# Earlier row loads, inverse matrices on semaphores of their own, and a reordered first wave in a spectral mixing and gated feed-forward kernel

## The reference

```python
X = np.fft.rfft(x, axis=1)                    # x: 4 x 3008 x 256
Yr = Xr @ w_r - Xi @ w_i + b_r
Yi = Xr @ w_i + Xi @ w_r + b_i
Yr, Yi = soft_threshold(Yr, 0.01), soft_threshold(Yi, 0.01)
y = np.fft.irfft(Yr + 1j * Yi, n=3008, axis=1)
h = y.reshape(12032, 256) @ w_in              # d_ff = 2048
P = a[0] + a[1]*h + a[2]*h**2 + a[3]*h**3
Q = 1 + abs(b[0])*abs(h) + abs(b[1])*h**2
out = (P / (Q + 1e-6)) @ w_out
```

## Time and profile before

| | us |
|---|---|
| median of 3 runs | 1527.56 |
| lowest and highest of them | 1527.35, 1531.04 |
| the profiled execution, its own time | 1528.65 |
| its span | 1526.9 |
| PE busy in the span | 1452.5 (95%) |
| DVE busy | 1273.0 (83%) |
| ACT busy | 1216.0 (80%) |
| POOL busy | 635.9 (42%) |

### The profile page before, as it was taken

One profiled execution on the slowest core, in us unless ns is written; L12 is line 12 of the kernel. 1 busy time (PEld: TensorE's weight loads), 2 busy tenths in 40 slices (PEclk: granted clock), 3 DMA queues, 4 the chain that ended last, 5 costly groups with the idle time before them and its releaser, 6 DMA issues.

```text
span 1526.9 us, 19941 instructions
## 1 busy us (share of the span) xinstructions
PE 1452.5 (95%) x6976; PEld 1231.3 (81%) x6976; DVE 1273.0 (83%) x1301; ACT 1216.0 (80%) x1577; POOL 635.9 (42%) x420
## 2 busy tenths in 40 slices
PE   6888999999999999999999999999999999999986
PEld 2666788888888888888888888888888778887775
DVE  0242888888888888889899899889999999999997
ACT  3454887888887887888888888888888888888886
POOL 0000344444444444444444444444455555555554
PEclk9999999999999999999999999999999999999999
DMA  8945565655655655555555564565455544555443
GB/s 262 285 131 153 106 141 114 151 127 122 137 129 111 145 128 114 133 112 115 111 125 102 116 128 94 115 128 114 88 120 113 102 89 102 110 107 101 95 78 69
DMA packets 97570, 187.90 MB, mean 123 GB/s; under 512 B 11104, under 2 KB 57504, under 8 KB 97472
## 3 DMA queue, kind: packets, MB, share of 16 engines
q0 software_dynamic: 29952, 98.58, 35.2%
q1 hardware_dynamic: 67520, 88.05, 20.0%
HBM read 50.54 MB, written 37.49 MB: 58 GB/s over the span
## 4 chain that ended last, share of the span: by engine, by line
PE 62%; DVE 21%; DMA 7%; issue 6%; ACT 2%; SPq 1%; POOL 1%; POOLq 0%; ACTq 0%
PE h_ps L359 20%; PE o_ps L372 7%; PE o_ps L384 7%; PE o_ps L374 7%; DVE num L642 5%; DVE g_hi L634 5%; DVE den L637 5%; DVE num L617 4%; PE d L332 4%; PE d L333 4%; DMA zp_in<-spec 3%; PE d L344 3%; PE d L338 2%; DMA inv_in<-in_inv 2%; PE d L319 2%
## 5 line engine op out<-in xcount | busy, mean ns | idle before, releaser
L661 POOL TENSOR_TENSOR g_lo<-num,sq 128x940 fp32r<-128x940 f32 (+1 forms) x208 | 453.5, 2180 | 260.5 <-DVE num L642 260.2
L652 POOL DMA_DIRECT2D den<-sq x208 | 182.5, 877 | 624.5 <-ACT sq L506 314.8
L372 PE MATMUL o_ps<-g_hi,wout_hi 128*128 128x470 f32 (+1 forms) x832 | 330.2, 398 | 0.0
L359 PE MATMUL h_ps<-yt_hi,win_hi 128*128 128x470 f32 (+1 forms) x832 | 312.5, 376 | 4.4 <-DVE num L622 3.0
L359 PE MATMUL h_ps<-yt_lo,win_hi 128*128 128x470 f32 (+1 forms) x832 | 312.0, 375 | 0.0
L359 PE MATMUL h_ps<-yt_hi,win_lo 128*128 128x470 f32 (+1 forms) x832 | 310.0, 373 | 0.0
L374 PE MATMUL o_ps<-g_hi,wout_lo 128*128 128x470 f32 (+1 forms) x832 | 309.1, 372 | 0.0
L384 PE MATMUL o_ps<-g_lo,wout_hi 128*128 128x470 f32 (+1 forms) x832 | 227.5, 395 | 30.1 <-POOL g_lo L661 29.9
L506 ACT ACTIVATE sq<-h_ps,bsq 128x940 f32<-128x940 f32 (+1 forms) x208 | 214.7, 1032 | 50.3 <-POOL g_lo L661 50.1
L503 ACT ACTIVATE den<-h_ps,b_sb 128x940 f32<-128x940 f32 (+1 forms) x208 | 213.8, 1028 | 48.3 <-PE h_ps L359 47.5
L642 DVE SCALAR_TENSOR_TENSOR num<-num,a_sb,den 128x940 f32<-128x940 f32 (+1 forms) x208 | 245.6, 1181 | 5.0
(11 more groups left out here) (64 smaller groups left out, 1492.1 us busy)
## 6 DMA issues: line engine op xcount, KB each, us to landing
den<-sq POOLq DMA_DIRECT2D x200, 470.0 KB, 4.4
xw<-in_x SPq DMA_DIRECT2D x32, 384.0 KB, 4.3
spec<-s1w SPq DMA_DIRECT2D x64, 192.0 KB, 3.3
z_in<-spec SPq DMA_DIRECT2D x96, 128.0 KB, 3.2
spec<-s_out SPq DMA_DIRECT2D x96, 128.0 KB, 3.3
out_t<-o_sb SPq DMA_DIRECT2D x25, 470.0 KB, 5.6
zp_in<-spec SPq DMA_DIRECT2D x22, 480.0 KB, 5.0
inv_in<-in_inv SPq DMA_DIRECT2D x96, 64.0 KB, 2.3
```

Of the source, the lines that this page charges most:

```text
L359: mm = pe.matmul(h_ps[q % 2][:, j, 0:cols(q)], w[:, h, f * P:(f + 1) * P], y[t % 2][:, h, 0:cols(q)], start=i == 0, stop=i == len(terms) - 1)
L372: pe.matmul(o_ps[:, h, 0:w], wout_hi[:, f, h * P:(h + 1) * P], g_hi[q % 2][:, j, 0:w], start=f == 0, stop=False)
L661: pool.tensor_tensor(g_lo[r % 2][:, :, 0:cols(r)], ring(num, r), ring(sq, r), ALU.mult).then_inc(n_g, 1)
```

## The change

It does six things.

1. `s_z` now counts row loads alone; the inverse matrices have semaphores `s_inv` of their own, on which s4 waits. `load_z` waits for `p2` (the s2 that last used the row buffer) in place of `p4`; a new `load_inv` waits for `p4`.
2. In the wave, SP at u loads the rows of step u+4 ahead of its stores (before: of step u+2, behind them), and the inverse of step u+2 behind its store.
3. In the start, the first x load is split in two halves with a semaphore `s_first` for the first half. The x loads 10 and 11, `fwd_sb` part 0, `wr_sb`, `wi_sb` and the bias no longer stand between the s1 stores; they come behind the 16th store, and the last three behind the first four row loads. PE waits for them at its first s3, not ahead of the wave.
4. The 12 s1 steps of batch 1 move from iterations 0 to 11 to the iterations in `EARLY_S1`, their x loads to `EARLY_X`.
5. The weight loads move from iterations 1 to 8 to every second one from 6 to 20; `weight_hi` and `weight_lo` start four iterations later.
6. s5 of tile 0 moves from behind the wave into iteration 27, its `group_f1(0)` into iteration 28, ahead of the last s4. `load_zp(1)` moves from slot 1 of the main loop to ahead of it. In the main loop the rows are loaded two slots earlier relative to their step.

```diff
+EARLY_S1 = {u: S1N + 4 + i for i, u in enumerate((4, 5, 7, 8, 9, 11, 12, 13, 15, 16, 17, 18))}
+EARLY_X = {u: S1N // 2 + 3 + i for i, u in enumerate((3, 5, 8, 11, 14))}
...
                 if c >= 4:
+                    sp.wait_ge(p2, c - 3)
+                load(z_in[c % 4][:, :], spec1[n, k2 * 4:(k2 + 1) * 4, :].rearrange("r (p d) -> (r p) d", d=D), s_z[c % 4])
+
+            def load_inv(c):
+                if c >= 4:
                     sp.wait_ge(p4, c - 3)
...
+                load(inv_in[c % 4][:, :], inv[c % K2], s_inv[c % 4])
...
+                if u < PRE and u + 4 < PRE + 4:
+                    load_z(u + 4)
...
                 if u >= 2:
                     store_s4(u - 2)
-                    if u + 2 < PRE + 4:
-                        load_z(u + 2)
-                if 1 <= u <= 8:
-                    load_weight(u - 1)
+                    load_inv(u + 2)
+                if u % 2 == 0 and 6 <= u < 22:
+                    load_weight(u // 2 - 3)
...
+                    if u == 1:
+                        pe.wait_ge(s_wc, 16 * 3)
...
+                if u == PRE - 1:
+                    pe.wait_ge(e1, 2 * S1N)
+                    pe.wait_ge(s_ff, 16)
+                    step_s5(0, o_ps[:, 0, :])
+                    step_s5(1, o_ps[:, 1, :])
+                if u == PRE:
+                    pe.wait_ge(w_lo, 8)
+                    pe.wait_ge(e2, 2 * PRE)
+                    group_f1(0)
```

More of the change, by code:

```diff
@@ L100, in z_slot @@
 def z_slot(c):
-    old = S2_SLOTS[c - 4 - PRE] + 3 if c - 4 >= PRE else 0
+    old = S2_SLOTS[c - 4 - PRE] + 1 if c - 4 >= PRE else 0
     n = c // K2
@@ L110 @@
     Z_AT.setdefault(z_slot(_c), []).append(_c)
+INV_AT = {(S2_SLOTS[_c - 4 - PRE] + 3 if _c - 4 >= PRE else 0): [] for _c in range(PRE + 4, NK)}
+for _c in range(PRE + 4, NK):
+    INV_AT[S2_SLOTS[_c - 4 - PRE] + 3 if _c - 4 >= PRE else 0].append(_c)
 def done_by(table, q, before):
@@ L163, in spectral_ffn @@
         s_w = [sem(f"s_w{i}") for i in range(8)]
+        s_first = sem("s_first")
         s_x = [sem(f"s_x{i}") for i in range(4)]
         s_z = [sem(f"s_z{i}") for i in range(4)]
+        s_inv = [sem(f"s_inv{i}") for i in range(4)]
         s_zp = [sem(f"s_zp{i}") for i in range(2)]
@@ L218, in load_z @@
                 if c >= 4:
+                    sp.wait_ge(p2, c - 3)
+                load(z_in[c % 4][:, :], spec1[n, k2 * 4:(k2 + 1) * 4, :].rearrange("r (p d) -> (r p) d", d=D), s_z[c % 4])
+            def load_inv(c):
+                if c >= 4:
                     sp.wait_ge(p4, c - 3)
-                load(z_in[c % 4][:, :], spec1[n, k2 * 4:(k2 + 1) * 4, :].rearrange("r (p d) -> (r p) d", d=D), s_z[c % 4])
-                load(inv_in[c % 4][:, :], inv[k2], s_z[c % 4])
+                load(inv_in[c % 4][:, :], inv[c % K2], s_inv[c % 4])
             def load_fwd(i):
@@ L259, in _ @@
             load(c1_sb[:, :], c1, s_tc)
-            load_x(0)
+            load(x_in[0][:, 0:2, :].rearrange("r p d -> r (p d)"), x[0, :, 0:2 * D], s_first)
+            load(x_in[0][:, 2:4, :].rearrange("r p d -> r (p d)"), x[0, :, 2 * D:4 * D], s_x[0])
             load(a_sb[:, :], coef_a, s_coef)
@@ L266, in _ @@
                 store_s1(g)
-                if g % 2 == 1:
+                if g % 2 == 1 and g // 2 + 4 < S1N // 2 + 2:
                     load_x(g // 2 + 4)
[L269 to L273, removed]
+            load_fwd(0)
             for c in range(4):
                 load_z(c)
-            for u in range(PRE + 2):
[L277 to L281, removed]
+            load(wr_sb[:, :, :], w_r.rearrange("(h p) e -> p h e", p=P), s_wc)
+            load(wi_sb[:, :, :], w_i.rearrange("(h p) e -> p h e", p=P), s_wc)
+            load(bias_sb[:, :], bias, s_wc)
+            load_inv(0)
+            load_inv(1)
+            load_x(S1N // 2 + 2)
+            load_inv(2)
+            load_inv(3)
+            for u in range(PRE + 2):
                 if u < 3:
@@ L285, in _ @@
                     load_zp(0)
+                if u < PRE and u + 4 < PRE + 4:
+                    load_z(u + 4)
+                if u == 0:
+                    for g in range(S1N, S1N + 4):
+                        store_s1(g)
+                if u - 1 in EARLY_S1:
+                    store_s1(EARLY_S1[u - 1])
+                if u in EARLY_X:
+                    load_x(EARLY_X[u])
                 if u >= 2:
                     store_s4(u - 2)
-                    if u + 2 < PRE + 4:
-                        load_z(u + 2)
-                if 1 <= u <= 8:
-                    load_weight(u - 1)
+                    load_inv(u + 2)
+                if u % 2 == 0 and 6 <= u < 22:
+                    load_weight(u // 2 - 3)
                 if u == 9:
                     load(c5_sb[:, :], c5, s_ff)
+            load_zp(1)
             for k in range(S1N, S1N + 4):
@@ L301, in _ @@
                     load_z(c)
+                for c in INV_AT.get(q, []):
+                    load_inv(c)
                 if q - 1 in S1_AT:
@@ L306, in _ @@
                         load_x(g // 2 + 4)
-                if q % SLOTS == 1 and q // SLOTS + 1 < NT:
+                if q % SLOTS == 1 and 1 <= q // SLOTS < NT - 1:
                     load_zp(q // SLOTS + 1)
@@ L316, in step_s1 @@
             def step_s1(g, bank):
-                pe.wait_ge(s_x[g // 2 % 4], (g // 8 + 1) * 16)
+                if g == 0:
+                    pe.wait_ge(s_first, 16)
+                else:
+                    pe.wait_ge(s_x[g // 2 % 4], (g // 8 + 1) * 16)
                 at = g % 2 * 2
@@ L322, in step_s2 @@
             def step_s2(c, bank):
-                pe.wait_ge(s_z[c % 4], (c // 4 + 1) * 32)
+                pe.wait_ge(s_z[c % 4], (c // 4 + 1) * 16)
                 for h in range(KH):
@@ L336, in step_s4 @@
             def step_s4(c, bank):
+                pe.wait_ge(s_inv[c % 4], (c // 4 + 1) * 16)
                 pe.wait_ge(m_thr, c + 1)
@@ L392, in _ @@
                 step_s1(g, o_ps[:, g % 2, :])
-            pe.wait_ge(s_wc, 16 * 3)
             for u in range(PRE + 2):
@@ L408, in _ @@
                     step_s4(u - 2, (d0, d1)[u % 2][:, :])
-                g = S1N + 4 + u
-                if g < 2 * S1N:
+                if u in EARLY_S1:
+                    g = EARLY_S1[u]
                     pe.wait_ge(e1, g - 1)
                     step_s1(g, o_ps[:, g % 2, :])
[L413 to L418, removed]
+                if u == PRE - 1:
[7 more added lines that the diff above has]
+                    group_f1(0)
             pe.wait_ge(m_t, PRE)
-            group_f1(0)
             group_f1(1)
@@ L521, in _ @@
                     below(u - 1)
-                g = S1N + 4 + u
-                if g < 2 * S1N:
+                if u in EARLY_S1:
+                    g = EARLY_S1[u]
                     evacuate_s1(g, o_ps[:, g % 2, :])
[L525 to L528, removed]
+                if 10 <= u < 26 and u % 2 == 0:
+                    weight_hi((u - 10) // 2)
+                if u == PRE - 1:
+                    evacuate_s5(0, o_ps[:, 0, :])
+                    evacuate_s5(1, o_ps[:, 1, :])
             act.wait_ge(w_lo, 8)
@@ L606, in _ @@
                 shifted(u - 1, h_ps[1][:, (u - 1) % 2, :])
-                if 7 <= u < 23 and u % 2 == 1:
-                    weight_lo((u - 7) // 2)
+                if 11 <= u < 27 and u % 2 == 1:
+                    weight_lo((u - 11) // 2)
                 soft(u - 1)
-            split_lo(0, o_ps[:, 0, :])
-            split_lo(1, o_ps[:, 1, :])
+                if u == PRE - 1:
+                    split_lo(0, o_ps[:, 0, :])
+                    split_lo(1, o_ps[:, 1, :])
             for q in range(NS + 1):
```

## The result

The changed kernel takes 1515.84 us (median of 5 runs, 1513.61 to 1518.10) against 1527.56 (by now the median of 5 runs too, 1526.08 to 1531.04): ratio 0.992, 95% interval 0.9903 to 0.9938. It is faster by 11.7 us where 21.8 were forecast, and lies outside the range of 1501 to 1513.

A forecast was written before the change was run, and what follows sets the result against it. The prediction took row reloads to bound the wave and the DMA queue the start. Start, wave and end terms put group 0 at 127.3 for 149.09, 21.8 us less: 1506.85 from 1528.65, about 1506 against the median; range 1501 to 1513.

The forecast's parts named there:

- From there both kernels run the same: ACT, DVE, then f1(2): From ACT's begin of group 0, forecast at 127.3 for 149.09 us, both kernels were to run the same.
- The main loop I cost at nothing: Main loop: rows go out in the same odd slots, PE's own matmuls hide them, so no time was added.
- s3(0) after 36: Start: a sign that the forecast is wrong, PE's first s3 coming after 36 us.
- First row load near 28: Start: a sign that the forecast is right, SP's first row load at 28.2 for 32.43 us.
- s3(0) at 33.7: Start: PE begins its first s3 at 33.7 for 38.42 us, bounds 33.1 to 35.9, a gain of 4.7 us.
- for completion: Start: some 0.7 us added after the queue has moved 1.57 MB by 32.8, giving 33.5 us.
- The wave: First s3 to the end of iteration 27: 79.9 us of PE work, plus 1.5 for cover and 2.6 for low clock.
- the 1.5 us for the short cover: Wave: the chain s3, bias, neg, ythr, s4 has one iteration of cover, nearly closed without an s1; 1.5 us (0 to 5).
- (b): Rival, wave: the DMA queue binds; some 22 MB at only 220 GB/s take 100 us, 10 more: 1516 us; chance 0.13.
- (c): Rival, wave: the row load was not the limit; only start and end gain, 4.7 and 1.7 us: 1521 us; chance 0.04.
- s5 late by 1.6: End of the wave: s5 waits 1.6 us (0 to 4) for zp_in, whose load waits for the store of s4(23).
- rival (a): Low clock stays: group_f1(0) takes 4.37 us, and a second s3 and a half run low: 1510 us; chance 0.11.

The follow-up runs named there:

- before_late_x2: The kernel before with load_zp(1) and x loads 16 to 19 made to wait for group_f1(0), some 2.6 us ahead of the first den DMA: 1535.31 us.
- x_half2: The changed kernel with x loads 18 and 19 (786 KB) moved from ahead of the main loop to its slots 2 and 3: 1513.52 us.
- x_zp2: The changed kernel with x loads 16 to 19 issued right behind load_zp(0) in iteration 26: 1507.93 us.
- tail_undone2: The changed kernel with s5 of tile 0 and group_f1(0) behind the whole wave again, SP's order unchanged: 1511.03 us.
- x_early2: The changed kernel with x loads 16 to 19 issued in iterations 21 to 24 of the wave instead of behind it: 1513.62 us.

## Why the prediction was wrong

The step that failed is "From there both kernels run the same: ACT, DVE, then f1(2)", with "The main loop I cost at nothing". They did not run the same: the first `den` DMA took 11.1 us for 4.5, and 6.5 us were lost behind group 0. Without them the 4.2 us by which group 0 was late would have left the time inside the range. Two of the signs named for a wrong forecast came: s3(0) after 36, and a main loop longer by more than 2 us. Point by point, for the profiled execution (1517.63 measured, 1506.85 forecast, 10.8 us apart):

- **First row load near 28: right**, 28.80.
- **s3(0) at 33.7: 36.48, 2.8 late**, and beyond the bound of 35.9. The first row load went out 0.6 us later than forecast (28.80 for 28.2), and so the bias, at 31.61. It then took 4.8 us to land, where the forecast left it 2.7 (from 31.0 to 33.7). In the four other profiles with this start s3(0) came at 33.65 to 34.66, near the forecast, but by luck: there the rows went out at 26.90 to 27.51, earlier than forecast, and the bias took 3.7 to 4.9 us. The term that was too small is the landing of the bias. Of its parts, the 0.7 us "for completion" stand in no row.
- **The wave: right.** From s3(0) to the end of iteration 27 it took 82.4 us for 84.0. The low clock behind the wait for the bias cost 2.8 us for 2.6 (from 36.48 to 41.1 the granted clock was 0.50), and the 1.5 us for the short cover were not needed. Without an s1 an iteration takes 2.60 us in the chain. s2 waited for rows once, 1.8 us, in iteration 0. The reload of the rows was the limit, and rivals (b) and (c) are refuted: the wave moved 232 GB/s and ran out of nothing.
- **s5 late by 1.6: 3.0 late**, since the store ahead took 2.67 us for the 1.78 between store and load in the earlier trace rows, and the load 4.68 for 4.3.
- **The low clock at the end, rival (a), came in part.** s5 took 3.01 for 2.22 at a granted clock of 0.78, and s3(27) with s4(26) 3.29 for 2.16 at 0.68, together 1.9 us more; `group_f1(0)` itself ran at 1.00, in 2.56. With all that, and 0.3 won at ACT's copy, group 0 began at 131.48 for 127.3, 4.2 late. Rival (c) gave the end of the wave 1.7 us, but the forecast's own terms make it 2.8 (149.09 - 136.73 against 127.3 - 117.7).
- **The rest: 1384.3 for 1377.8 us, 6.5 lost.** 4.2 and 6.5 are the 10.7 of the spans.

What the runs showed in the place of the failed step: the order of PE decides when SP's queue is let go. I had followed the waiting store on SP and asked who needs the loads behind it ("needed two slots later"), but not which other DMA is in flight when they all go at once. The cause is shown from three sides. Put into the kernel before, where nothing else changes, it costs 6.0 us by slot 4 (before_late_x2). Fewer bytes shorten `den` in step, 11.1, 7.9 and 4.8 us for 2.06, 1.28 and 0.49 MB issued just ahead of it or beside it (changed, x_half2, x_zp2). And taken out by moving four loads, it gives back 7.9 us of median (x_zp2); in the profiles the rest gives 7.4.

The Trainium skill has the rule, on the page "DMA: Bandwidth & Descriptors", section "Issuing engines are not separate DMA queues": DMAs started by SP and by GpSimd run on the same 16 engines and interleave. The trace agrees: POOL's DMA took 11.1 us while SP's five loads moved, and 4.5 without them.

As for the parts: 1 and 2 alone bring 17.6 us. Part 6 (s5 and f1 inside the wave) is worth about 3 us when no collision stands in the way: 1507.93 with it (x_zp2) against 1511.03 without it (tail_undone2), whose x loads do not collide either. The two also differ in where the x loads stand. The forecast had given the end of the wave about 2.8. In the change as made, part 6 brought the collision and cost 4.8 us net. Parts 3, 4 and 5 together brought nothing that could be told apart: 1511.03 with them and without part 6, 1510.42 without. Their gain at s3(0), 4.5 us in the profiles, was there, and in tail_undone2 it was spent again. 2.2 us went in the wave (82.6 for 80.4), which began at a granted clock of 0.50 after a wait of 3.3 us for the bias. 2.5 us went at its end, where the last s4 waited 2.3 us behind a late store and s5 ran 4.42 us for 3.08, at a granted clock of 0.50. Whether part 5 alone does anything was not tried.

## What to carry to other kernels

When a wait is moved on an in-order queue, list everything queued behind it that will be let go together, and ask what else is in flight at that moment on the shared DMA engines; here an x load that s1 used 21 us after its issue helped to cost 6 us by its company. Read a chain's loop first: here one edit of a wait and of the order of two loads gave 17.6 us, more than all six parts together. And sum a forecast beyond the stage that was changed, through the first steps of the next one, where both the clock and the queues still carry what the stage left behind.

## What was not expected of the hardware

- A 470 KB accumulating DMA of POOL (4.5 us) took 11.1 us when SP put out 2.06 MB from 1.6 us ahead of it on. In that stretch the engines were full at about 240 GB/s (134 to 146 us: share 1.02, 243 GB/s), and the late DMA finished about when all the bytes had moved; its being issued by another engine did not protect it.
- The same start took 1.8 to 2.8 us more in one profile than in four others: s3(0) at 36.48 for 33.65 to 34.66. Two things vary: when the last s1 store has landed, so that the first row load went out at 28.80 for 26.90 to 27.51, and the time of the bias from issue to landing, 3.7 to 4.9 us.
- After a wait of 6.2 us the 20 short matmul records of s5 took 4.55 us for 2.22 (x_early2), at a granted clock of 0.50, the lower of the two levels; the s3 and s4 behind them had 0.56, and `group_f1(0)` had 1.00. In the changed kernel, after a wait of 2.8 us, the same three had 0.78, 0.68 and 1.00.
